# Four small edits to a three-stage kernel: one split in the first attention iteration, two GpSimd drains, one register load, and the place of a block of transposes

## What is computed

```python
# attention: batch 4, 8 heads, 768 positions, head size 64, 4 sinks, window 128
scores = scale * np.matmul(q, k.transpose(0, 1, 3, 2))
keep = is_sink | in_window
scores = np.where(keep, scores, -1000000000.0)
a = softmax(scores); attn_out = np.matmul(a, v)
x = attn_out.transpose(0, 2, 1, 3).reshape(3072, 512)
# dense: 512 -> 2048 -> 512
h = x @ w_in
x = (h * np.cos(h)) @ w_out
# experts: 8 of 512 -> 1024 -> 512
logits = x @ w_gate + modality_bias[modality_id]
e_idx = np.argmax(logits, axis=1)
for e in range(E):
    h = np.maximum(x[mask] @ w1[e], 0.0)
    out[mask] = gate_w[mask, None] * (h @ w2[e])
```

## Time and profile before

| quantity | value |
|---|---|
| runs | 1059.81, 1059.84, 1059.86 us |
| the profiled execution's own time | 1059.81 us |
| its span in the trace | 1058.1 us |
| TensorE matmul busy | 1048.3 us, 99% of the span |
| VectorE, ScalarE, GpSimd busy | 678.5, 468.3, 283.4 us |
| granted TensorE clock | 1.00 over the whole span |
| attention, dense layer, experts | to about 204, 204 to 743, 743 to 1058 us |

### The profile page before, as it was taken

One profiled execution on the slowest core, in us unless ns is written; L12 is line 12 of the kernel. 1 busy time (PEld: TensorE's weight loads), 2 busy tenths in 40 slices (PEclk: granted clock), 3 DMA queues, 4 the chain that ended last, 5 costly groups with the idle time before them and its releaser, 6 DMA issues.

```text
span 1058.1 us, 18467 instructions
## 1 busy us (share of the span) xinstructions
PE 1048.3 (99%) x5870; PEld 900.8 (85%) x5871; DVE 678.5 (64%) x1503; ACT 468.3 (44%) x975; POOL 283.4 (27%) x374
## 2 busy tenths in 40 slices
PE   8999999999999999999999999999999999999998
PEld 8999999888888888888888887888988998899996
DVE  7899999866687568758857767976852223522222
ACT  6888888755433343343333335335442212422212
POOL 6888888501000000000000000431332222322222
PEclk9999999999999999999999999999999999999999
DMA  6677788525220020002002001002372111311100
GB/s 199 204 214 216 199 255 261 181 80 161 80 80 1 1 69 12 1 0 80 1 1 81 1 1 39 6 22 81 127 267 69 57 37 44 112 51 60 39 20 21
DMA packets 57358, 90.72 MB, mean 86 GB/s; under 512 B 11470, under 2 KB 40526, under 8 KB 57168
## 3 DMA queue, kind: packets, MB, share of 16 engines
q1 hardware_dynamic: 50816, 75.17, 22.4%
q0 software_dynamic: 6208, 14.40, 4.2%
q10 hardware_dynamic: 272, 0.39, 0.2%
HBM read 70.86 MB, written 21.69 MB: 87 GB/s over the span
## 4 chain that ended last, share of the span: by engine, by line
PE 93%; POOL 3%; DMA 1%; issue 1%; DVE 1%; ACT 0%; POOLq 0%; SPq 0%; DVEq 0%; ACTq 0%
PE twin L1845 25%; PE bank L1895 13%; PE twin L1895 13%; PE twin L1967 12%; PE twin L1982 12%; PE bank L1767 6%; PE bank L1746 2%; PE twin L1734 2%; PE twin L1733 2%; PE bank L1774 2%; POOL k_lo L655 1%; PE bank L1933 1%; PE twin L2008 1%; POOL qs L657 1%; PE bank L1784 1%
## 5 line engine op out<-in xcount | busy, mean ns | idle before, releaser
L726 POOL DMA_INDIRECT list_scratch<-entry,slot_i x24 | 26.8, 1117 | 472.2 <-DVE slot_i L1480 460.9
L1845 PE MATMUL twin<-x_hi,w_hi 128*128 128x512 f32 x380 | 151.1, 398 | 0.0
L1845 PE MATMUL twin<-x_hi,w_lo 128*128 128x512 f32 x380 | 150.4, 396 | 0.0
L1845 PE MATMUL twin<-x_lo,w_hi 128*128 128x512 f32 x380 | 150.3, 396 | 0.0
L1967 PE MATMUL twin<-xg_both,w_hi 128*128 128x256 f32 x768 | 140.1, 282 | 0.3 <-DVE xg_both L1506 0.2
L1606 DVE SCALAR_TENSOR_TENSOR g_lo<-twin,g_hi 128x256 fp32r<-128x256 f32 x96 | 40.7, 424 | 145.5 <-ACT g_hi L1036 145.2
L1967 PEld LDWEIGHTS twin<-xg_both,w_hi 128*128 128x128 f32 x768 | 121.9, 188 | 6.9 <-issue 0.7
L1000 ACT ACTIVATE turns<-turns 128x512 f32<-128x512 f32 x96 | 60.8, 633 | 131.9 <-DVE turns L1383 131.9
L1365 DVE CUSTOM_DVE_ANT_0 whole<-y_sb,raw 128x512 f32<-128x512 f32 x160 | 109.9, 687 | 1.9
L992 ACT ACTIVATE turns<-twin 128x512 f32<-128x512 f32 x95 | 56.4, 593 | 117.4 <-PE twin L1845 117.3
L1967 PE MATMUL twin<-xg_both,w_lo 128*128 128x256 f32 x384 | 107.2, 279 | 0.0
(11 more groups left out here) (246 smaller groups left out, 2423.5 us busy)
## 6 DMA issues: line engine op xcount, KB each, us to landing
raw<-w_expert SPq DMA_DIRECT2D x24, 512.0 KB, 4.5
raw_q<-q_twice SPq DMA_DIRECT2D x31, 384.0 KB, 3.8
raw<-w_dense SPq DMA_DIRECT2D x16, 512.0 KB, 4.5
raw_k<-k_twice SPq DMA_DIRECT2D x16, 448.0 KB, 3.8
raw_k<-k_twice SPq DMA_DIRECT2D x16, 416.0 KB, 4.8
v_sb<-v_n SPq DMA_DIRECT2D x16, 384.0 KB, 4.2
xT_scratch<-x_stage SPq DMA_DIRECT2D x16, 384.0 KB, 3.8
x_raw<-xT_scratch SPq DMA_DIRECT2D x6, 1024.0 KB, 5.5
```

The source lines that it names most:

```text
L1845: last = pe.matmul(hidden_bank(c, f)[:, :], a[:, w], b[:, k, :], start=k == 0 and x == 0, stop=k == KD - 1 and x == 2)
```

## The change

1. The second row of `FIRST_PARTS` goes. In iteration 0 the steps n = 6 to 11 now follow `PARTS`, so ScalarE splits part 3 (k, second half) of the following pair behind step 10 and not behind step 11.
2. Both `pool.drain()` between `rows_back` and `free_rows` go.
3. On ScalarE, VectorE and TensorE the load of `n_turns` moves from ahead of tile 1 to behind the first expert's last tile, ahead of the loop that uses it.
4. In a tail tile that is not alone, `turn_rows(t + 1)` moves from ahead of the wait for the first down product to between down products 4 and 5 (f counted from 0; 3 of the 8 stand behind it).

```diff
-        FIRST_PARTS = ((), (0,), (1,), (2,), (), (3,)), ((0,), (), (1,), (2,), (), (3,))
+        FIRST_PARTS = ((), (0,), (1,), (2,), (), (3,))
...
             rows_back(1)
-            pool.drain()
             free_rows(1)
...
                 rows_back(t + 1)
-                pool.drain()
                 free_rows(t + 1)
...
-                        for c in (FIRST_PARTS[n // QB] if isinstance(it, int) and it == 0 else PARTS)[n % QB]:
+                        for c in (FIRST_PARTS if isinstance(it, int) and it == 0 and n < QB else PARTS)[n % QB]:
...
-            n_turns = act.value_load(table[0:1, T_TURNS:T_TURNS + 1], min_val=1, max_val=NE // 2)
             n_used = act.value_load(table[0:1, T_USED:T_USED + 1], min_val=1, max_val=NE)
             _, last, whole_end = turn_of(mybir.EngineType.Activation, 0)
             tiles_of(1, whole_end, last, 0, 0)
+            n_turns = act.value_load(table[0:1, T_TURNS:T_TURNS + 1], min_val=1, max_val=NE // 2)
             with act.Fori(0, n_turns) as rr:
...
                 tail_hidden(1, base, range(1, KD)).then_inc(eh_done, 2)
-                if not alone:
-                    turn_rows(t + 1, ET_BANK)
                 pe.wait_ge(h_lo_made, n + 5)
                 tail_down(t, 0, base, r)
...
-                for f in range(4, FB2):
+                for f in range(4, FB2 - 3):
+                    tail_down(t, f, base, r)
+                if not alone:
+                    turn_rows(t + 1, ET_BANK)
+                for f in range(FB2 - 3, FB2):
                     tail_down(t, f, base, r)
```

More of the change, by code:

```diff
@@ L1702, in tiles_of @@
                         tail_tile(whole_end)
-            n_turns = dve.value_load(table[0:1, T_TURNS:T_TURNS + 1], min_val=1, max_val=NE // 2)
             n_used = dve.value_load(table[0:1, T_USED:T_USED + 1], min_val=1, max_val=NE)
@@ L1707, in _ @@
             tiles_of(1, whole_end, last, 0, 0)
+            n_turns = dve.value_load(table[0:1, T_TURNS:T_TURNS + 1], min_val=1, max_val=NE // 2)
             with dve.Fori(0, n_turns) as rr:
@@ L2083, in _ @@
             pe.wait_ge(table_made, 1)
-            n_turns = pe.value_load(table[0:1, T_TURNS:T_TURNS + 1], min_val=1, max_val=NE // 2)
             _, last_tile, whole_end = turn_of(mybir.EngineType.PE, 0)
             expert_tiles(1, whole_end, last_tile, 0, 0)
+            n_turns = pe.value_load(table[0:1, T_TURNS:T_TURNS + 1], min_val=1, max_val=NE // 2)
             with pe.Fori(0, n_turns) as rr:
```

## The result

| | before | after |
|---|---|---|
| median of the runs compared | 1059.53 us (6 runs, 1059.10 to 1059.86) | 1068.95 us (6 runs, 1068.79 to 1069.55) |
| span of the profiled execution | 1058.1 us | 1067.2 us |
| the profiled execution's own time | 1059.81 us | 1068.91 us |

The ratio is 1.0090, with a 95% interval of 1.0078 to 1.0103: 0.9% slower, about 9.4 us. The prediction had 1061.4 us and a range up to 1062.3. It was wrong, in size and in its likeliest outcome (no change).

What follows compares the result with a forecast made beforehand. The prediction took TensorE, busy 99% of the span, as the bound. Its terms, +0.25 + 0 - 0.28 + 0.6 + 0.98 = +1.55 us, took 1059.81 to 1061.36, predicted as 1061.4 us, range 1060.2 to 1062.3.

Steps and rivals of the forecast that it cites:

- likeliest outcome (no change): Whole kernel: time within 0.2%, 2.1 us, of before; chance 0.81.
- Part 2, "So 0": GpSimd's loop drains, 4.06 us each: removing them changes the time by 0, since what comes earlier waits for TensorE anyway.
- Part 1, +0.25: Attention, split at step 10: a new stall costs 1.0 us, the later one's 0.76 goes, net +0.25.
- the stall at 32.86: Attention: ScalarE's earlier split waits 1.16 us for GpSimd's fill, making TensorE's transposes about 1.0 us late.
- The stall at 44: Attention, fourth pair: ScalarE's 0.94 us wait for GpSimd's fill vanishes, giving back 0.76 us on TensorE.
- the slower rival: Attention: GpSimd's fill is late too, deciding from 0.6 us, so the later stall stays; sum 2.3, time 1062.1; chance 0.09.
- Part 3, -0.28 and +0.6: Moved `n_turns` load on ScalarE: -0.28 us at tile 1's third block, +0.6 at tile 7's third block.
- Part 4, +0.98: Tail tile 6: transposes paid again between down products, +0.87 us, and first down product 0.11 later, +0.98 together.
- the wait for g_lo: Tail tile's first down product: without transposes filling VectorE's wait, it begins at 895.11 instead of 895.00, +0.11 us.
- The instruction fetch: Rival at tile boundaries: a branch waits for its code, idling TensorE a few us; time 1063; chance 0.06.
- the faster rival: GpSimd's drains hold something unseen, such as output buffers; removal saves 2 to 4 us, 1057.4 to 1059.4; chance 0.04.
- The figure of the Trainium skill: Register load behind the tail tile: about 1.3 us by the page in place of 0.6, raising the sum by 0.7.

## Why the prediction was wrong, point by point

**Part 2, "So 0": this step failed.** It asked who waits for a drain, found that nobody does, and took its removal as free. It even put a limit on its error: "one drain would cost or give at most 4 us; nothing in the rows comes near". Both sentences treat a drain's 4.06 us as a cost of that place only. The runs show that part of it is work owed for each software DMA, 0.082 us, which a later drain has to do if this one doesn't. The later drain is the one at the program's end, where no engine covers it. The term was 96 more DMAs by 0.082 = 7.9 us (98 more with the two fills), on the path that sets the end. Had the 7.86 of the trace been in the sum, 1061.36 + 7.86 = 1069.2 would have stood beside the measured 1068.95. The end drain was not in the rows that the prediction rests on, though the kernel before has it: 220 ns behind 2 DMAs, beside later ones of 4.06 behind 5 and a first one of 9.9 us behind 38:

```profile
L822 POOLq DRAIN  x1: 9905/9905/9905, 777.0 to 777.0; - x1
```

That a drain's length goes with the number of DMAs ahead of it could have been asked from these.

**Part 1, +0.25.** The mechanism was right: the stall at 32.86 is 1.22 (1.16 forecast), and the transposes are at 34.96 (34.98 forecast). The stall at 44 did not vanish; 0.31 is left, because the fill comes 0.4 to 0.5 later. That is the mechanism of the slower rival, which needed 0.6 to decide, at part of its strength. In the changed kernel the net is +0.41 behind pair four.

**Part 3, -0.28 and +0.6.** At tile 1 the gap is gone; the shift against the kernel before goes from +0.13 at the tile's start to -0.05 at the third block's first matmul and -0.16 behind it, so -0.29 in all. At tile 7 it goes from 0.69 at the start to 1.25 at the third block, +0.56. Both are as forecast, in place, sign and size. In the changed kernel VectorE's and TensorE's moved loads show no wait.

**Part 4, +0.98.** The tail tile costs 0.81: the shift at tile 7's first matmul is 901.75 - 901.06 = 0.69, from -0.12 in the hidden products of the tail tile. The transposes are paid again with 0.82 (0.87 forecast). What was too high is the wait for g_lo: the first down product begins at 894.87, 0.13 earlier than before, which is no later than the tile itself runs, where 0.11 later was forecast. From the end of VectorE's g_lo to it are 0.24 us, in place of 0.33.

**The sum without part 2.** Behind tile 7's third block TensorE is 1.25 late in the changed kernel and 1.79 in the one with the drains put back; 1.55 was forecast. The two differ by drift and not by a part: the dense layer begins 0.41 and 0.74 late, and on the way into tile 1, where no part acts, they gain 0.28 and 0.10. The parts read one by one in the changed kernel give +0.41 - 0.29 + 0.56 + 0.81 = 1.49.

**The rivals.** The instruction fetch did not show: behind the first microseconds TensorE's longest wait in the changed kernel is 0.7 us. The faster rival named the drains, and had the sign wrong. No rival had them cost time. The third outcome, a cost moved to where nothing covers it, was missing from the list.

The figure of the Trainium skill weighed in part 3 (page "Runtime: NRT & Kernel Launch"; it stands in the section "The launch sequence") is one for loads from HBM. It does not carry over to this load from SBUF: tile 7 lost 0.56, not 1.3. On drains the Trainium skill has one sentence that bears on this: page "VectorE: DVE Perf Modes", section "The DRAIN you can't avoid", says that the runtime's own drains, ahead of and behind a kernel, are a constant of about 12 ns on all engines. Whether it means the end drains seen here is not shown. If it does, the trace agrees for TensorE (8 ns) and SyncE (13 ns), and not for ScalarE (304 ns), VectorE (455 ns) and above all GpSimd (220 to 8076 ns).

## What to carry to other kernels

When a synchronizing instruction is removed because nobody waits for it, ask also what it does for the instructions ahead of it, and who does that once it is gone. Here that was the drain at the program's end, which is never hidden. Look at the last microseconds of the span by themselves, sequencers included: the page's busy times and chain showed nothing of an 8 us instruction. And a drain can be rare, but it should be late: one drain of 9.3 us at tile 11, under TensorE's work, did nearly the work of thirteen (1060.65 us against 1059.71), and the end pays 0.082 us for each software DMA behind the last drain.

## What the runs showed of the hardware that was not expected

GpSimd's end drain lasts 0.082 us for each software DMA issued since its last drain, from 2 of them (0.22 us) to 62 (5.13 us), and 8.08 us for 100, and it does so when every transfer has landed: in the changed kernel GpSimd had waited for the scatters of each tile before it went on, and for the last ones before the end drain. In the loop the same instruction lasts 4.06 us for 5 DMAs, but in the tile shown GpSimd is only 0.33 us faster without it. Whether the price goes by DMAs or by rows, and what GpSimd does in that time, no run here shows.
